# Transposing raw q and k together, and moving the sum of an output's halves to ScalarE and GpSimd

## What is computed

```python
# attention: q, k, v are (2, 8, 768, 64), proj is (64, 6)
q_bits, k_bits = (q @ proj > 0), (k @ proj > 0)
mask = (bucket(q_bits)[:, :, :, None] == bucket(k_bits)[:, :, None, :])
scores = where(mask, (q @ k.T) / sqrt(64), -1e9)
attn = exp(scores - max(scores)); attn = attn / (sum(attn) + 1e-9)
x = (attn @ v), heads side by side            # (1536, 512)
# gated MLP: w1, w2 (512, 1024), w3 (1024, 1024), w_out (1024, 512)
x = ((x @ w1) * (x @ w2)) @ w3 @ w_out
# mixture: four experts e, p = domain_probs / their sum
out = sum over e of p[:, e] * (relu(x @ w1[e]) @ w2[e])
```

## Time and profile before

| | |
|---|---|
| median of 3 runs | 992.93 us (992.86 to 993.02) |
| the profiled execution | 992.96 us, of which 991.2 us are the span |
| TensorE busy, with its weight loads beside it | 984.3 us (99%), 917.4 us (93%) |
| VectorE, ScalarE, GpSimd busy | 626.4, 464.3, 436.7 us |
| granted TensorE clock | 1.00 in every stretch |
| attention loop | from about 67 to 307 us, 15.06 us per head in its middle |

### The profile page before, as it was taken

The page is one execution under the profiler, slowest core; times in us unless marked ns, Lnnn a source line. Parts: engine busy times, 40 slices in busy tenths (PEclk is TensorE's granted clock), DMA queues, the critical chain, the costliest instruction groups (busy, mean ns, idle before and its releaser), DMA issues.

```text
span 991.2 us, 15991 instructions
## 1 busy us (share of the span) xinstructions
PE 984.3 (99%) x5494; PEld 917.4 (93%) x5494; DVE 626.4 (63%) x964; ACT 464.3 (47%) x853; POOL 436.7 (44%) x446
## 2 busy tenths in 40 slices
PE   9999999999999999999999999999999999999998
PEld 7889999999989999999998998989989899898997
DVE  6359999999997995598755352544535545355342
ACT  4248888888875543555542340422404224042230
POOL 4024445367797991694263160431604316043130
PEclk9999999999999999999999999999999999999999
DMA  6223333232233220101100111001110011010102
GB/s 245 88 65 89 90 103 87 80 107 86 70 84 93 64 64 22 43 22 43 44 22 22 55 31 43 22 22 50 37 36 29 21 45 40 31 32 21 43 22 105
DMA packets 57646, 57.44 MB, mean 58 GB/s; under 512 B 7552, under 2 KB 46592, under 8 KB 57600
## 3 DMA queue, kind: packets, MB, share of 16 engines
q1 hardware_dynamic: 57600, 56.85, 19.2%
HBM read 44.20 MB, written 3.19 MB: 48 GB/s over the span
## 4 chain that ended last, share of the span: by engine, by line
PE 98%; DVE 1%; ACT 0%; issue 0%
PE ps L291 24%; PE ps L292 24%; PE ps L293 24%; PE ps L1423 6%; PE ps L1410 3%; PE ps L1438 3%; PE ps L1412 3%; PE ps L1440 3%; PE ps L1373 2%; PE ps L1390 1%; PE ps L1332 1%; PE ps L1379 1%; PE ps L1325 1%; PE ps L1382 1%; DVE pT_lo L1024 0%; DVE expo L1006 0%
## 5 line engine op out<-in xcount | busy, mean ns | idle before, releaser
L636 POOL TENSOR_TENSOR v_sum<-kept,kept 128x384 f32<-128x384 f32 x48 | 51.8, 1080 | 287.3 <-ACT kept L822 287.3
L822 ACT COPY kept<-ps 128x384 f32<-128x384 f32 x144 | 67.7, 479 | 206.4 <-PE ps L293 205.4
L1300 DVE SCALAR_TENSOR_TENSOR acc<-ps,gate,acc 128x512 f32<-128x512 f32 x96 | 72.0, 750 | 139.5 <-PE ps L293 139.5
L293 PE MATMUL ps<-v_hi,hid_lo 128*128 128x512 f32 x384 | 149.6, 390 | 0.0
L292 PE MATMUL ps<-v_lo,hid_hi 128*128 128x512 f32 x384 | 149.5, 389 | 0.0
L291 PE MATMUL ps<-v_hi,hid_hi 128*128 128x512 f32 x384 | 149.4, 389 | 0.0
L1006 DVE TENSOR_SCALAR_CACHE_REDUCE expo<-ps 128x768 f32<-128x768 f32 x96 | 91.7, 956 | 14.2 <-PE ps L1412 10.6
L724 ACT ACTIVATE expo<-expo,neg_max 128x768 f32<-128x768 f32 x96 | 90.7, 945 | 5.9 <-DVE expo L1006 4.5
L1024 DVE TENSOR_TENSOR pT_lo<-ps,pT_hi 128x768 fp32r<-128x768 f32 x96 | 90.5, 947 | 1.6 <-ACT pT_hi L732 1.1
L1149 DVE TENSOR_TENSOR u_sum<-ps,kept 128x384 f32<-128x384 f32 x48 | 26.6, 554 | 100.5 <-PE ps L293 100.5
L732 ACT CAST pT_hi<-ps 128x768 fp32r<-128x768 f32 x96 | 76.9, 804 | 24.2 <-PE ps L1423 23.9
(11 more groups left out here) (164 smaller groups left out, 2529.6 us busy)
## 6 DMA issues: line engine op xcount, KB each, us to landing
w_raw<-in_moe_w SPq DMA_DIRECT2D x64, 128.0 KB, 2.4
e_raw<-in_moe_w SPq DMA_DIRECT2D x64, 128.0 KB, 2.4
v_raw<-in_moe_w SPq DMA_DIRECT2D x32, 256.0 KB, 3.1
w_raw<-in_moe_w SPq DMA_DIRECT2D x8, 512.0 KB, 3.7
raw_q<-in_q SPq DMA_DIRECT2D x16, 192.0 KB, 2.6
raw_k<-in_k SPq DMA_DIRECT2D x16, 192.0 KB, 2.6
raw_v<-in_v SPq DMA_DIRECT2D x16, 192.0 KB, 2.7
k_main<-k_cross SPq DMA_DIRECT2D x16, 192.0 KB, 2.7
```

Source lines behind the costliest of these rows:

```text
L293: return nc.tensor.matmul(out_ps, lhs_lo, rhs_hi, start=False, stop=stop, skip_group_check=onto)
L636: nc.gpsimd.tensor_tensor(v_sum[:, :], kept[s][1][:, :], kept[s][2][:, :], ALU.add).then_inc(v_done, 1)
L822: nc.scalar.copy(kept[s][n][:, :], ps[4 * s + n][:, 0:HALF]).then_inc(kept_done, 1)
L1300: nc.vector.scalar_tensor_tensor(acc[:, t, :], ps[4 * ((h + t // 4) % 2) + t % 4], gate_f[:, bass.ds(t * E + e, 1)], acc[:, t, :], ALU.mul ...
```

## The change

1. **q and k are loaded beside each other** in one tile `raw_qk`, whose row holds q's 64 values and then k's. Six raw 128x128 transposes (steps 0 and 1) bring both to `qk_T`, q in rows 0 to 63 and k in rows 64 to 127. Before, there were twelve, of parts. A head has 5 steps instead of 7.
2. **The split comes after the transposes**: ScalarE makes two copies per head instead of four, and GpSimd (`split_qk`) one cast to `q_main` and one subtraction to `q_cross`, both 128x768, in place of four operations of 128x384 and two of 64x768.
3. **More is moved by SyncE**: the high part of k to two places and its low part to one (`move_k`), then, once these have landed and the projection is done, the high part of q to `q_cross` (`move_q`). The one-hot moves are as before.
4. **An output's halves**: ScalarE copies the high rows straight to `x_raw` and the low rows to `o_low` (`o_copy`), and GpSimd adds them per pair of heads, 128x384 twice, ahead of its two multiplications. VectorE's `o_sum` is gone. ScalarE's copy to `o_low` for an even head waits until GpSimd has scaled the pair before.

The diff, cut to its core:

```diff
-    GROUPS = 7
+    GROUPS = 5
+
+    FIRST_STEPS = (0, 1, None, None, 2, 3, 4)
...
-        raw_q = [place(f"raw_q{s}", [P, TILES, DH], F32, prep_at) for s in range(2)]
-        raw_k = [place(f"raw_k{s}", [P, TILES, DH], F32, prep_at) for s in range(2)]
-        q_parts = [place(f"q_parts{s}", [P, TILES, P], F32R, prep_at) for s in range(2)]
-        k_parts = [place(f"k_parts{s}", [P, TILES, P], F32R, prep_at) for s in range(2)]
-        proj_w = [place(f"proj_w{n}", [P, P], F32R, prep_at) for n in range(6)]
+        raw_qk = [place(f"raw_qk{s}", [P, TILES, 2, DH], F32, prep_at) for s in range(2)]
+        qk_T = [place(f"qk_T{s}", [P, S], F32, prep_at) for s in range(2)]
+        proj_hi = [place(f"proj_hi{h}", [P, P], F32R, prep_at) for h in range(2)]
+        proj_lo = [place(f"proj_lo{h}", [P, P], F32R, prep_at) for h in range(2)]
...
+        def first_step(n):
+            return FIRST_STEPS[n % len(FIRST_STEPS)]
...
-                    sp.wait_ge(k_split, 2 * i + s - 1)
-                for raw, heads in ((raw_q, q_heads), (raw_k, k_heads)):
-                    sp.dma_start(raw[s][:, :, :].rearrange("p t d -> p (t d)"), heads[2 * i + s, :, :])\
+                    sp.wait_ge(prep_mm, GROUPS * (2 * i + s - 2) + 2)
+                for n, heads in enumerate((q_heads, k_heads)):
+                    sp.dma_start(raw_qk[s][:, :, n, :], heads[2 * i + s, :, :].rearrange("p (t d) -> p t d", d=DH))\
                         .then_inc(qk_loaded[s], 16)
...
+            def move_k(m, s):
+
+                sp.wait_ge(qk_hi_done, m + 1)
+                move(parts_moved[s], (k_main[s][0:DH, :], q_main[s][DH:P, :]), (k_cross[s][0:DH, :], q_main[s][DH:P, :]))
+                sp.wait_ge(qk_split, m + 1)
+                move(parts_moved[s], (k_cross[s][DH:P, :], q_cross[s][DH:P, :]))
+
+            def move_q(m, i, s):
+
+                sp.wait_ge(parts_moved[s], 48 * (i + 1))
+                sp.sem_inc(sp_held, 1)
+                sp.wait_ge(prep_mm, GROUPS * m + 3)
+                move(stacks_moved[s], (q_cross[s][DH:P, :], q_main[s][0:DH, :]))
...
-                    move_high(2 * i + 2 + s, s)
+                    move_k(2 * i + 2 + s, s)
                     if not last:
                         load_qk(i + 2, s, False)
                     spread_reciprocals(2 * i + s, i, s, first)
+                    move_q(2 * i + 2 + s, i + 1, s)
...
-            def split_q(m, i, s, first):
-
-                if not first:
-                    pool.wait_ge(prep_mm, GROUPS * (m - 2) + 4)
-                pool.wait_ge(qk_loaded[s], 32 * (i + 1))
+            def split_qk(m, s):
+
+
+                pool.wait_ge(prep_copied, 2 * m + 2)
                 held()
-                nc.gpsimd.tensor_copy(q_parts[s][:, :, 0:DH], raw_q[s][:, :, :]).then_inc(q_hi_done, 1)
-                pool.wait_ge(q_hi_done, m + 1)
-                nc.gpsimd.tensor_tensor(q_parts[s][:, :, DH:P], raw_q[s][:, :, :],
-                                        q_parts[s][:, :, 0:DH].bitcast(F32), ALU.subtract).then_inc(q_split, 1)
-
-            def split_k(m, s):
-
-                nc.gpsimd.tensor_copy(k_parts[s][:, :, DH:P], raw_k[s][:, :, :]).then_inc(k_hi_done, 1)
-                pool.wait_ge(k_hi_done, m + 1)
-                nc.gpsimd.tensor_tensor(k_parts[s][:, :, 0:DH], raw_k[s][:, :, :],
-                                        k_parts[s][:, :, DH:P].bitcast(F32), ALU.subtract).then_inc(k_split, 1)
-
-            def stack_highs(m, s, values):
-
-
-                pool.wait_ge(v_split, values)
-                for part, (rows, src) in enumerate(((slice(0, DH), q_cross), (slice(DH, P), k_cross))):
-                    pool.wait_ge(prep_copied, 4 * m + 2 * part + 2)
-                    held()
-                    nc.gpsimd.tensor_copy(q_main[s][rows, :], src[s][rows, :].bitcast(F32)).then_inc(highs_stacked, 1)
-                    pool.wait_ge(highs_stacked, 2 * m + part + 1)
+                nc.gpsimd.tensor_copy(q_main[s][:, :], qk_T[s][:, :]).then_inc(qk_hi_done, 1)
+                pool.wait_ge(qk_hi_done, m + 1)
                 held()
+                nc.gpsimd.tensor_tensor(q_cross[s][:, :], qk_T[s][:, :], q_main[s][:, :].bitcast(F32), ALU.subtract)\
+                    .then_inc(qk_split, 1)
...
+                cols = slice(hf * HALF, (hf + 1) * HALF)
+                x = x_raw_f[:, bass.ds(i * S + hf * HALF, HALF)]
+                pool.wait_ge(o_copied, 8 * i + 4 + 2 * hf + 2)
+                held()
+                nc.gpsimd.tensor_tensor(x, x, o_low[:, cols], ALU.add).then_inc(x_added, 1)
                 pool.wait_ge(rec_spread, 32 * i + 32)
+                pool.wait_ge(x_added, 2 * i + hf + 1)
                 held()
-                x = x_raw_f[:, bass.ds(i * S + hf * HALF, HALF)].rearrange("r (t p) -> r t p", p=P)
+                x = x.rearrange("r (t p) -> r t p", p=P)
                 nc.gpsimd.tensor_tensor(x, x, rec_cols[:, hf * HT:(hf + 1) * HT, :], ALU.mult).then_inc(x_scaled, 1)
...
-                        split_q(m + 2, i + 1, s, False)
-                        split_k(m + 2, s)
+                        split_qk(m + 2, s)
                     if s == 0:
                         split_v(m + 1, i, 1, first)
                     elif not last:
                         split_v(m + 1, i + 1, 0, False)
-                    if not last:
-                        stack_highs(m + 2, s, m + 2)
                     if s == 0 and not first:
                         x_scale(i - 1, 0)
                         x_scale(i - 1, 1)
...
-                dst = (q_cross if j < 2 else k_cross)[s]
-                half = slice((j % 2) * HALF, (j % 2 + 1) * HALF)
-                nc.scalar.copy(dst[:, half], ps_prep[:, 0:HALF]).then_inc(prep_copied, 1)
+                nc.scalar.copy(qk_T[s][:, j * HALF:(j + 1) * HALF], ps_prep[:, 0:HALF]).then_inc(prep_copied, 1)
...
-            def o_lower(n, bank):
+            def o_copy(n, i, s, hf, bank, first):
+
+                rows = slice(s * DH, (s + 1) * DH)
                 act.wait_ge(pv_mm, n + 1)
-                nc.scalar.copy(o_low[:, :], bank[DH:P, 0:HALF]).then_inc(o_low_done, 1)
+                nc.scalar.copy(x_raw_f[rows, bass.ds(i * S + hf * HALF, HALF)], bank[0:DH, 0:HALF]).then_inc(o_copied, 1)
+                if not first and s + hf == 0:
+                    act.wait_ge(x_scaled, 2 * i)
+                nc.scalar.copy(o_low[rows, hf * HALF:(hf + 1) * HALF], bank[DH:P, 0:HALF]).then_inc(o_copied, 1)
...
                     copy(2, 1)
                     exp(0, 5)
-                    copy(2, 2)
                     lower(-1, 1)
                     if first and s == 0:
                         wp_high(FK - 1)
                     pT_high(6 * m + 3, 3)
-                    copy(2, 3)
                     pT_high(6 * m + 4, 4)
                     exp(1, 0)
...
-            def o_sum(n, i, s, hf, bank):
-
-                dve.wait_ge(o_low_done, n + 1)
-                nc.vector.tensor_tensor(x_raw_f[s * DH:(s + 1) * DH, bass.ds(i * S + hf * HALF, HALF)],
-                                        bank[0:DH, 0:HALF], o_low[:, :], ALU.add).then_inc(o_full_done, 1)
...
-                    encode(1, 5)
+                    encode(1, 3)
                     scale(0, 3)
-                    add_parts(-1, 0)
-                    encode(1, 6)
+                    encode(1, 4)
                     scale(0, 4)
                     pT_low(6 * m + 0, 0)
                     scale(0, 5)
                     pT_low(6 * m + 1, 1)
                     pT_low(6 * m + 2, 2)
                     scale(1, 0)
-                    add_parts(-1, 1)
...
+                blocks = [(h, slice(n * DH, (n + 1) * DH), slice(c, c + BITS))
+                          for h in range(2) for n, c in enumerate((h * DH, h * DH + KBIT))]
+                for h, rows, cols in blocks:
+                    nc.vector.tensor_copy(proj_hi[h][rows, cols], proj_f[rows, :]).then_inc(proj_hi_ready, 1)
...
-            def prep(m, s, j, first):
-
+            def prep(m, i, s, j, first):
 
                 if j == 0 and not first:
                     pe.wait_ge(prep_coded, 3 * m)
-                elif 1 <= j < 4:
-                    pe.wait_ge(prep_copied, 4 * m + j)
-                elif j > 4:
-                    pe.wait_ge(prep_coded, 3 * m + j - 4)
+                elif j == 1:
+                    pe.wait_ge(prep_copied, 2 * m + 1)
+                elif j > 2:
+                    pe.wait_ge(prep_coded, 3 * m + j - 2)
                 if j == 0:
-                    pe.wait_ge(q_split, m + 1)
-                if j == 2:
-                    pe.wait_ge(k_split, m + 1)
-                if j < 4:
-                    parts = (q_parts if j < 2 else k_parts)[s]
+                    pe.wait_ge(qk_loaded[s], 32 * (i + 1))
+                if j < 2:
+
                     for tt in range(HT):
-                        last = nc.tensor.transpose(ps_prep[:, tt * P:(tt + 1) * P],
```

(55 more changed lines are left out.)

88 lines of the change are left out of this document (36 added, 52 removed).

## The result

The changed kernel takes 1000.79 us (median of 4 runs, 1000.36 to 1002.54) against 992.97 us for the one before (992.86 to 993.04) beside it: a ratio of 1.0081, with a 95% interval of 1.0067 to 1.0095. It is slower, as forecast, but by 7.8 us and not by 2.3, and it lies outside the range of 989.5 to 998.5. The profiled execution took 1001.16 us, its span 999.4 (before 991.2).

The account below looks back on a forecast made before the run. It took TensorE, 99% busy, as the bound, with a ScalarE and VectorE chain practically tied. Terms: -1.3 (heads 0 and 1), +1.3 (loop), +2.3 (end of attention) = +2.3 us, giving 995.2 us; range 989.5 to 998.5.

Parts of the forecast that it names:

- The chain beside TensorE: ScalarE and VectorE steps in each head, ending some 0.04 us before TensorE needs them; practically tied with TensorE.
- T5: Last transposes of exponentials in a head on TensorE (198.07); forecast to wait for the fourth tile's low part.
- S2: Next head's third score tile on TensorE, waiting for VectorE's scaling of the second; forecast about 198.75 instead of 198.65.
- The guard: VectorE's tiny 128x6 instruction on the row sums; forecast to wait for GpSimd's subtraction, about 1.3 us in 14 heads.
- ScalarE's cast: Cast of the fourth transposed tile of exponentials; forecast to stay near 195.88, behind two copies as before.
- B: Transposes of the second q half on TensorE (192.97); the next come at 208.03, a head of 15.06 us.
- ScalarE's wait for `o_low`: ScalarE's second output copy in even heads waits 0.6 us until the pair before is scaled; absorbed, price 0.
- The first rival: TensorE is the bound throughout, so nearly all removed transpose groups count: -7.6 us, 985.3 us; chance 0.12.
- That is +0.1 us per head: Attention loop: the guard's wait delays the fourth tile's subtraction; +0.1 us instead of -0.66, times 14, +1.4 us.
- TensorE's first gate products move by +2.3 us: End of attention: two adds lengthen GpSimd's scaling of a pair, delaying the first gate weights; bounds 1.8 to 3.
- The last rival: A new wait once per pair: GpSimd's adds take 1.7 us instead of 1.02; 1002.6 us, chance 0.13.
- SyncE at price 0: Three more moves per head and a wait for landing fit SyncE's idle time; 7 us if 0.5 late per head.

Follow-up runs that it names:

- e7_three: Changed kernel with output halves as before the change, no guard instruction, and SyncE's read-back of the reciprocals behind the one-hot moves: 987.61 us.
- e1_no_guard: Changed kernel without VectorE's guard instruction, reciprocals taken of the row sums themselves: 998.56 us.
- e13_guard_acc: e10_four with the guard and its addition of 1e-9 back, in a form that also accumulates the least value: 986.71 us.
- e12_halves_only: Kernel before the change, with only the output halves copied twice by ScalarE and added by GpSimd: 1007.81 us.
- e4_fill: Changed kernel with 14 thrown-away 128x384 matmuls on TensorE in its wait ahead of the first gate product: 999.42 us.
- e10_four: e7_three with GpSimd's combinations for the third gate weights ahead of the last pair's scaling: 985.51 us.
- e9_combine_first: Changed kernel with GpSimd's combinations for the third gate weights ahead of the last pair's adds and multiplications: 998.13 us.
- e8_guard_tt: Changed kernel with the guard written as a sum of two tiles instead of a tile and a number: 1003.25 us in one run.
- e5_joint_no_guard: Changed kernel with output halves as before the change and no guard instruction: 990.20 us.

## Why the prediction was right in sign and wrong in size

**Right.** The chain beside TensorE: the removed transposes bought nothing in the loop, TensorE waits at T5 and S2 instead. The guard lasts 1.25 us in the middle of its 16 instances, forecast about 1.3. ScalarE's cast has not moved (2.97 and 2.83 us after B in odd and even heads, 2.91 before). ScalarE's wait for `o_low` was forecast at 0.6 us and is 0.59, absorbed. The projection's operands were in time. GpSimd's pair at the end grew by 2.4 us, forecast 2.3, and TensorE waits 2.74 us for the first gate weights, forecast about 3. The idle time in the loop is smaller in the table of waits than forecast (5.8 us, not some 10): the profile counts it from the modelled end of the matmul before, and at T5 its 0.45 us stand for 0.78 from start to start, where 0.175 is usual. The first rival (TensorE the bound, 985.3 us) needed the chain to be 0.55 us shorter; in e7_three its heads are 0.45 us shorter, and 5.9 us show between the first and the last B (190.09 us for 195.94).

**A term mis-sized: the guard.** "That is +0.1 us per head". It is 0.22: 0.18 from B to S2 and 0.04 from there to the next B. GpSimd's subtraction ends 4.04 us after B instead of 3.93: the cast starts 1.20 after B (I had 1.13 there, and 1.16 in the sum for the end of attention), and the subtraction 1.00 after the cast, not 0.90. In the row that I had taken that interval from the earlier trace rows the profile shows no wait between the two, though the program has one there as well; here it shows 0.18 us, and why the two rows differ is open. Over 13 heads the loop lost 3.0 us instead of 1.3. That the wait is the guard's is shown by e1_no_guard (15.10 us in the undisturbed heads) and e13_guard_acc, where a guard that does not wait leaves heads of 14.61 to 14.69 us, all but the first; e12_halves_only fits.

**The steps that failed: what follows the adds.** "TensorE's first gate products move by +2.3 us", and there the sum stopped. That term itself is right (2.63 measured). Two terms behind it are missing, that is, they stood at nothing without a reason, and they alone carry the time out of the range.

The wait itself has a price beyond its length: TensorE, idle for 2.74 us, came back at a granted clock of 0.50, and the next 3.7 us of work cost 1.3 us more (e4_fill: 1.4). A wait of 1.2 us at the same place, in e10_four, cost no clock (1.00 from 280 to 300). The fall does not seem to come in every run: one of the four runs of the changed kernel, one of five of e1_no_guard and two of six of e9_combine_first have a mean clock of 1.000 instead of 0.998, but no trace of such a run is there.

And the last pair has the same two adds. I priced them once, for the pair before the last. Behind the last pair's scaling GpSimd combines the third gate weights, and TensorE's next steps depend on these: 2.3 us by the traces, 2.7 (or 1.8, see there) by e9_combine_first. Together 3.6 us; with them and the guard's true size the forecast's own sum is 995.2 + 1.7 + 3.6 = 1000.5, next to 1000.8.

The last rival (1002.6) came nearer than the forecast by luck. Its mechanism did not occur: GpSimd's adds in the attention stage took 1.00 to 1.02 us, not 1.7, and the pairs brought no new wait into the loop.

**Not quite right: SyncE at price 0.** In the changed kernel's trace it holds, for TensorE waits 1.8 us for one-hot moves in four heads and these are no longer than the others; in the trace of e8_guard_tt, with eight such waits, the loop is 1.1 us longer. It held because the guard cost more. "Late one-hot moves" was a side remark in the last rival; it should have been a step, since the read-back of the reciprocals waits for GpSimd's scaling, which the adds move by 2.4 us, with the one-hot moves behind it in the queue.

**The parts are not additive.** The joint transposes alone cost 5.1 us (2.3 in the traced run, the only one that the account of their waits covers) and the halves alone 14.8, both together 7.8. The explanation that fits, from the traces: the k copy that the one removes makes room for the copy that the other adds; without that room a head takes 15.5 us (e12_halves_only).

The Trainium skill, page "SBUF — State Buffer", section "Who interferes with whom", says that a VectorE instruction with two SBUF inputs contends with a GpSimd instruction that reads SBUF, that `tensor_scalar` can take the shared ports in its 2-port modes, but not the form that also writes out its accumulator, and that the wait lasts for the whole instruction. e8_guard_tt (0.99 us in the middle), the changed kernel's guard (1.25) and e13_guard_acc (0.15) agree.

## What to carry to other kernels

Where TensorE is busy 99%, still measure how late the next chain arrives at the points where it waits at all: 0.04 us of slack made the 9.2 us of matmuls that were saved in the loop worth nothing. When work is added to an engine, follow its queue to every place where the loop leaves it, the last iteration too, and ask after each new wait what stands behind it in the queue and whether TensorE's clock outlasts it. A tiny instruction can be the costliest of a head; its form decides.

## What the hardware showed that I had not expected

- The 128x6 guard takes 0.15 us while GpSimd's subtraction is in flight if it accumulates as well (e13_guard_acc), and up to 1.6 us in the forms without that. The reciprocal of the same size takes 0.18 us in all kernels, also at 199.58 of the changed one, with GpSimd's add (199.40 to 200.40) in flight.
- After 2.7 us of idle time the granted clock of TensorE was 0.50, back at 1.00 by 305.5; after 1.2 us (e10_four) it did not fall. It fell in all seven traces with a wait of 2.40 to 3.05 us at this place.
- Most of the experiments' kernels scatter more from run to run (988.3 to 991.4 us in e5_joint_no_guard, 986.4 to 989.1 in e7_three) than the one before (992.2 to 993.2 beside them). The waits for one-hot moves alone do not explain it, for e7_three has only one, of 0.2 us, and e4_fill has five and scatters by 0.3 us. The cause is open.
